# Attention with mixture of experts: the value products of a step in one group, with VectorE's and ScalarE's work around them moved

## The reference, cut to what matters

```python
def _attn_ref(q, k, v, n_sink, window):          # (2, 8, 768, 64) each, n_sink 4, window 128
    scores = scale * np.matmul(q, k.transpose(0, 1, 3, 2))
    keep = is_sink | in_window                   # 4 first keys, and the last 128 before each query
    scores = np.where(keep, scores, -1000000000.0)
    scores = scores - np.max(scores, axis=-1, keepdims=True)
    a = np.exp(scores)
    a = a / (np.sum(a, axis=-1, keepdims=True) + 1e-09)
    return np.matmul(a, v).astype(np.float32)

attn_out = _attn_ref(...)
x = attn_out.transpose(0, 2, 1, 3).reshape(B * S, H * D)   # 1536 x 512
x = _moe_ref(x=x, ...)      # each token to one of 8 experts, 192 per expert; relu(x @ w1) @ w2
return _moe2_ref(x=x, ...)  # x @ w_in, leaky relu with alpha, @ w_out
```

## Time and profile before

| | before |
|---|---|
| median of 3 runs | 635.64 us (635.63 to 636.36) |
| the profiled execution | 635.48 us, span 633.6 us |
| TensorE busy | 614.9 us (97%) |
| VectorE busy | 418.6 us (66%) |
| ScalarE busy | 308.5 us (49%) |
| GpSimd busy | 196.5 us (31%) |
| granted TensorE clock, mean of the span | 0.996 |
| the twelve attention steps until the first instruction of the routing | until 111.04 us |

### The profile page before, as it was taken

How to read it: one execution, slowest core, us unless ns; L and a number is a source line. 1 busy time by engine, 2 the same in 40 slices (tenths; PEclk the granted TensorE clock), 3 DMA queues, 4 the chain that set the end, 5 groups by cost and what they waited for, 6 DMA issues and landing times.

```text
span 633.6 us, 12921 instructions
## 1 busy us (share of the span) xinstructions
PE 614.9 (97%) x4942; PEld 554.5 (88%) x4947; DVE 418.6 (66%) x1156; ACT 308.5 (49%) x716; POOL 196.5 (31%) x211
## 2 busy tenths in 40 slices
PE   8799999889999999999999999999999999999996
PEld 4689998759899888899999888999988989999995
DVE  7788887988576979844759797439687520035552
ACT  5888884512132655532236554322566542346663
POOL 5998881010121342111113421201233410113331
PEclk9999999899999999999999999999999999999999
DMA  7477754535450242037003510360017610000001
GB/s 261 152 260 273 276 192 161 190 96 198 140 204 1 68 171 104 2 114 264 14 2 103 204 37 2 137 254 1 2 67 246 243 64 13 1 1 1 1 1 50
DMA packets 31220, 72.36 MB, mean 114 GB/s; under 512 B 2876, under 2 KB 2936, under 8 KB 31160
## 3 DMA queue, kind: packets, MB, share of 16 engines
q1 hardware_dynamic: 27232, 60.69, 27.2%
q0 software_dynamic: 1984, 6.29, 3.0%
q10 hardware_dynamic: 1944, 4.56, 1.9%
HBM read 65.22 MB, written 6.32 MB: 113 GB/s over the span
## 4 chain that ended last, share of the span: by engine, by line
PE 78%; DVE 2%; issue 0%; ACT 0%; POOLq 0%; POOL 0%; DVEq 0%
PE bank L1602 22%; PE bank L1617 21%; PE bank L1514 14%; PE bank L1505 14%; PE bank L1392 3%; PE bank L1483 1%; PE bank L1461 1%; DVE beats L971 1%; DVE beats L942 0%; PE bank L1418 0%; PE bank L1445 0%; PE bank L1233 0%; PE bank L1438 0%; PE bank L1394 0%; DVE in_slot L1055 0%
## 5 line engine op out<-in xcount | busy, mean ns | idle before, releaser
L603 POOL TENSOR_TENSOR wi_lo<-w_in,wi_hi 128x512 fp32r<-128x512 f32 x64 | 89.0, 1392 | 272.5 <-ACT wi_hi L744 272.5
L942 DVE TENSOR_SCALAR beats<-rank_row,key 128x512 bf16<-128x512 f32 (+11 forms) x144 | 92.6, 664 | 11.5 <-PE bank L1394 11.5
L1617 PE MATMUL bank<-wo_lo,g_hi 128*128 128x512 f32 x192 | 76.0, 396 | 0.0
L1617 PE MATMUL bank<-wo_hi,g_lo 128*128 128x512 f32 x192 | 75.7, 394 | 0.0
L1617 PE MATMUL bank<-wo_hi,g_hi 128*128 128x512 f32 x192 | 75.5, 393 | 0.0
L1215 DVE SCALAR_TENSOR_TENSOR g<-bank,g_neg 128x384 f32<-128x384 f32 x64 | 35.5, 555 | 52.8 <-ACT g_neg L796 52.8
L794 ACT ACTIVATE g_neg<-bank 128x384 f32<-128x384 f32 x64 | 31.4, 491 | 78.1 <-PE bank L1602 77.7
L1602 PE MATMUL bank<-y_hi,wi_hi 128*128 128x384 f32 x256 | 57.9, 347 | 0.0
L770 ACT ACTIVATE h_t<-bank 128x192 f32<-128x192 f32 x64 | 21.2, 331 | 72.8 <-PE bank L1505 72.8
L670 ACT ACTIVATE prob<-neg_s,neg_max 128x260 f32<-128x260 f32 x96 | 48.8, 509 | 15.0 <-DVE neg_max L853 12.9
L1602 PE MATMUL bank<-y_lo,wi_hi 128*128 128x384 f32 x256 | 55.2, 336 | 0.0
(11 more groups left out here) (180 smaller groups left out, 1359.6 us busy)
## 6 DMA issues: line engine op xcount, KB each, us to landing
w_a<-moe_w SPq DMA_DIRECT2D x8, 1024.0 KB, 5.1
w_a<-moe_w SPq DMA_DIRECT2D x4, 2048.0 KB, 10.3
w_b<-moe_w SPq DMA_DIRECT2D x8, 1024.0 KB, 5.1
w_b<-moe_w SPq DMA_DIRECT2D x4, 2048.0 KB, 10.2
k_raw<-k_t SPq DMA_DIRECT2D x11, 512.0 KB, 5.3
q_raw<-q_t SPq DMA_DIRECT2D x11, 512.0 KB, 4.0
w_in<-moe_w_in SPq DMA_DIRECT2D x8, 512.0 KB, 5.0
w_out<-moe_w_out SPq DMA_DIRECT2D x8, 512.0 KB, 4.5
```

Source lines behind the costliest of these rows:

```text
L603: nc.gpsimd.tensor_tensor(out=wi_lo[:, f % 2, :, :], in0=w_in[:, :, f * P:(f + 1) * P], in1=wi_hi[:, f % 2, :, :].bitcast(F32), op=ALU.sub ...
L942: return nc.vector.tensor_scalar(out=beats[:, c % 3, lo:hi], in0=rank_row[:, lo:hi], scalar1=key[:, c:c + 1], scalar2=None, op0=op)
L1617: last = nc.tensor.matmul(DOWN_BANK[t][:, :], a[:, f % 3, t * P:(t + 1) * P], w[:, f % 2, :], start=(f == 0 and n == 0), stop=(f == FC - 1 ...
```

## The change

On TensorE the products of pairs 0 and 1 no longer stand at h = 7 of a slot: all four pairs of `end` are multiplied at h = 1. On VectorE the first half of `normalise`, with the sum of the logits, moves from h = 0 to h = 1, behind the second head's maximum, and the reciprocal of the sums moves from h = 2 to h = 1. Both now stand ahead of the copy of pair 0. On ScalarE `round_next_k(front + 1)` moves from the head of the slot to behind the second exponential.

```diff
--- before.py
+++ after.py
@@ -659,8 +659,6 @@
             def attention_slot(s):
                 front, mid, end = s, s - 1, s - 2
                 for h in range(H):
-                    if h == 0 and 1 < front + 1 < STEPS:
-                        round_next_k(front + 1)
                     if front < STEPS:
                         b = front % 2
                         act.wait_ge(maxed, H * front + h + 1)
@@ -670,6 +668,8 @@
                         nc.scalar.activation(prob[b][:, h, :], neg_s[:, h % 4, :], ACT.Exp,
                                              bias=neg_max[b][:, h:h + 1], scale=-1.0,
                                              accum_out=p_sum[b][:, h, 0:1]).then_inc(exped, 1)
+                    if h == 1 and 1 < front + 1 < STEPS:
+                        round_next_k(front + 1)
                     if h == 1 and 0 <= end < STEPS:
                         act.wait_ge(pv_done, 4 * (end + 1))
                         if end:
@@ -869,7 +869,7 @@
                         if i:
                             dve.wait_ge(x_stored[b], 16 * i)
                         normalise(end, 1).then_inc(halves_read, 1)
-                    if h == 0 and 0 <= late < STEPS:
+                    if h == 1 and 0 <= late < STEPS:
                         b, i = step(late)
                         dve.wait_ge(turned, 2 * late + 2)
                         chain.after(normalise(late, 0))
@@ -877,7 +877,7 @@
                                                 axis=AX, op=ALU.add).then_inc(x_ready, 1)
                     if 0 <= mid < STEPS:
                         b, i = step(mid)
-                        if h == 2:
+                        if h == 1:
                             dve.wait_ge(exped, H * (mid + 1))
                             chain.after(nc.vector.tensor_reduce(out=p_add[:, :], in_=p_sum[b][:, :, :], axis=AX, op=ALU.add))
                             nc.vector.reciprocal(p_inv[b][:, :], p_add[:, :]).then_inc(sums_read, 1)
@@ -1345,8 +1345,8 @@
                     elif front < STEPS:
                         keep_clock(5 if h == H // 2 - 1 else 1, OT_BANK)
                     if h == 1 and 0 <= end < STEPS:
-                        values(end, 2)
-                        values(end, 3)
+                        for r in range(PAIRS):
+                            values(end, r)
                     if h == sinks_at(mid) and 0 <= mid < STEPS:
                         turn_sinks(mid)
                     if h == 4 and 0 <= end < STEPS:
@@ -1355,9 +1355,6 @@
                         sink_values(mid)
                     if h == 6 and 0 <= end < STEPS:
                         turn_and_gate(end, 0)
-                    if h == 7 and 0 <= mid < STEPS:
-                        values(mid, 0)
-                        values(mid, 1)
 
             pe.wait_ge(zeros_ready, 1)
             keep_clock(19, PT_BANK[0])
```

## The result

| | before | changed |
|---|---|---|
| median | 635.63 us (634.56 to 636.36, 4 runs) | 642.09 us (640.63 to 642.45, 4 runs) |
| ratio | | 1.0099, 95% interval 1.0077 to 1.012 |
| profiled execution | 635.48 us, span 633.6 | 640.63 us, span 638.9 |
| first instruction of the routing (L923) | 111.04 us | 116.50 us |

The change makes the kernel slower, by 6.5 us where 3.5 were forecast. The profiled execution is the fastest of the four, 1.5 us under their median. In the profiled pair all of the loss lies ahead of the routing: from L923 to the end of the span it is 522.6 us before and 522.4 after.

A forecast was written before the change was run, and what follows sets the result against it. TensorE was taken to bound slots 4 to 10; late keys would make GpSimd's chain the bound. Delays over the slots plus 0.51 at the end gave 3.63 us, so 635.48 became 639.11, forecast 639.1, range 638.0 to 640.6.

The forecast's parts named there:

- What bounds the kernel now: Slots 4 to 10: TensorE alone sets 7.61 us a slot; the rounded keys have 1.86 us of slack.
- The value products: TensorE: two of four gaps per slot go, saving 0.34 us, so its own work falls from 7.61 to 7.27.
- The rounded keys, and what follows on GpSimd: Keys end 2.19 us later, L366 starts at 3.14, next slot at 8.04 us; each slot grows by 0.43.
- VectorE, and the queues behind the waits: Moved VectorE pieces lose nothing, pair 0's copy ends at about 3.2 us; queued ScalarE and SyncE work shifts along.
- The sum for slots 2 to 4: Slot 2 starts as before at 24.54, slot 3 at +0.31, slot 4 at 40.75, +0.08 us.
- The end: Slots 11 and 12: slot 11 takes 0.34 less, slot 12's 16 products add 0.85, together +0.51 us.
- the one in which the keys are covered: Rival: L366 starts by 2.37, TensorE stays the bound, about 1.9 us saved, 633.6 us; chance 0.07.
- GpSimd was not stretched: Rival: the late start also stretches GpSimd, +0.6 us in each of eight slots, 644 us; chance 0.07.
- Nothing was made up behind the attention: Rival: the loss is made up behind the attention by a transfer as late anyway, 635.7 us; chance 0.04.

The follow-up runs named there:

- keys_back: Changed kernel with ScalarE rounding the next step's keys at the head of the slot again: 635.55 us, ratio 0.999 to the kernel before.
- group_only: Kernel before with only TensorE's value products of a step put in one group: 636.49 us, ratio 1.0008.
- keys_after_first: Changed kernel with the keys rounded behind the first exponential of a slot instead of the second: 637.81 us, ratio 1.0035 to the kernel before.
- keys_only: Kernel before with only ScalarE's rounding of the keys moved behind the second exponential: 645.29 us, ratio 1.0135.
- slot1_filled: Changed kernel with 19 unused products of zeros on TensorE in slot 1's waits: 640.79 us, ratio 1.0079 to the kernel before.
- the second (642.10 and 636.77): Changed kernel unaltered, timed again (6 runs) against 11 runs of the kernel before: 642.1 us, ratio 1.0082.
- before_look2: Third trace of the kernel before, nothing changed, taken to look for falls of TensorE's clock; L923 at 110.92 us.
- change_look3: Fourth trace of the changed kernel, nothing altered, taken for the place of the clock's fall; L923 at 115.32 us.
- change_look2: Third trace of the changed kernel, nothing altered, taken for the place of the clock's fall; L923 at 115.90 us.
- keys_back_filler: Changed kernel with keys rounded at the head of the slot and five products of zeros in slot 1: 635.71 us, ratio 0.9984 to the kernel before.
- keys_back_look: Second trace of the changed kernel with keys rounded at the head of the slot; L923 at 112.88 us.

## Why the prediction was wrong in size

*What bounds the kernel now*: right. TensorE sets 7.61 us in slots 4 to 10, and the keys had 1.86 us of slack, too little for a move by 2.19.

*The value products*: the term of 0.34 us a slot was right. It shows wherever the keys are early (7.27 block to block in keys_back and group_only).

*The rounded keys, and what follows on GpSimd*: right in mechanism and nearly in size. L366 came at 3.18 to 3.28 into a slot, and a slot took 8.10 on average for 8.04 forecast. The term was too small by 0.06 us, over seven slots 0.41. In slot 6 it lies in two hand-overs: the first maximum starts 0.64 after the slot's first load, not 0.55, and L366 starts 0.13 behind the end of the keys, not 0.06. The whole of the growth is tied to the keys' place by keys_back, keys_after_first and keys_only.

*VectorE, and the queues behind the waits*: right. The copy of pair 0 ended 3.07 us into a slot that began at 58.37, 3.2 was the bound, and no one on TensorE waited for it:

```profile
60.79 0.65 DVE L893 COPY prob_t<-bank 128x512 f32<-128x512 f32 x1
```

*The sum for slots 2 to 4* is the step that failed: it had slot 4 at 40.75, and it started at 42.11, 1.36 later. It let TensorE's work in slot 2 run as before ("Slot 2 starts as before", "Slot 4 at 40.75, against 40.67: +0.08"). It never asked what slot 1 looks like without its value products, though TensorE idled there for long already. The half clock in slot 2 is 0.97 of the 1.36, by slot1_filled. The rows that I had cited for the clock said only that it was full before, and I took that as given for the changed kernel. Another 0.13 is the execution's later start (24.67 for 24.54). The last 0.26 was an error in the sum that the trace of the kernel before could have shown: at full clock slots 2 and 3 take 16.47, the sum had 16.21. For the mask of slot 2 I took the 3.22 us of slot 4 from the end of L359 to the next L366. In slot 2 itself it is 3.47, before as in slot1_filled (32.64 to 36.11):

```profile
29.94 2.37 POOL L359 TENSOR_TENSOR q_hl<-q_raw,q_hl 64x1024 fp32r<-64x1024 f32 x1
...
35.78 2.39 POOL L366 TENSOR_TENSOR k_lo<-k_raw,k_hi 128x1024 fp32r<-128x1024 f32 x1
```

*The end*: +0.57 measured, +0.51 forecast.

Together, in the profiled pair: 1.44 + 3.45 + 0.57 = 5.46 us until L923, against 0.08 + 3.04 + 0.51 = 3.63. Without the fall and the later start it is 4.35 (101.15 against 96.80), so the sum was 0.7 too small even at full clock. The measured medians lie 6.5 us apart in the first comparison and 5.3 in the second (642.10 and 636.77). The difference between these two I take for scatter of both kernels; the last section shows where the traces scatter, but no trace is of the slower three of the first four runs. The range was too narrow for this scatter: I had built it from the chain's terms, and from three runs that lay within 0.7 us by luck.

*The rivals*: the one in which the keys are covered needed L366 by 2.37; it started at 3.2. GpSimd was not stretched (L366 2.38 us). Nothing was made up behind the attention. The Trainium skill (TensorEngine Tiling (Array Packing), Key Properties) has TensorE drained at a change of tiling mode. The traces agree in the place, with gaps of 0.17 us around each block, and merging two blocks removes two of them; that the gaps are the drain is not shown apart from their place, and they had no say in the changed kernel's time.

## What to carry to other kernels

Before moving a small piece behind waits, follow what it feeds to the end: here 1 us of work on ScalarE started a chain of 4.9 us on GpSimd, and the slack of that chain, 1.86 us, could be read from three rows. A saving on the bounding engine is worth only what the second-slowest chain leaves: with early keys GpSimd took back 0.4 us in every second slot, until its own start was moved. Work taken out of a stretch in which TensorE already idles may cost its clock; look there as well as at the path. And where one execution differs from the next by a microsecond, measure from a place behind the difference: from slot 1 to L923 traces of one program with the same clock agree to 0.03 us.

## What the runs showed of the hardware

Half clock came in stretches of 3.4 us, or twice that, and not at the same place in each execution of the same program: between 17 and 20 us in two traces of the changed kernel, between 26 and 29 in the other two. Behind the attention each trace has at least one.

Much of the scatter of all versions comes together with a late one. before_look2 had half clock from 145 to 149 us, where the first expert's products begin, and took 524.5 us from L923 to the end, where the first trace, at full clock there, took 522.6. (It had one more stretch, at 128 to 131 us; change_look3, with two stretches ahead of 140 us but none from there to 160, took 523.0.) Its stretches (144 to 148, 148 to 152), then those of the first trace:

```profile
144.00:148.00 4.00, 4.00 (x50) 3.83 (x51) 4.00 (x9) 0.91 (x3) 0.00 (x0) 0.67 1.05 398
148.00:152.00 4.00, 4.00 (x56) 3.87 (x55) 2.57 (x6) 0.66 (x2) 0.00 (x0) 0.90 0.86 322
```

```profile
144.00:148.00 4.00, 4.00 (x57) 3.87 (x54) 4.00 (x10) 0.83 (x3) 0.00 (x0) 1.00 1.01 387
148.00:152.00 4.00, 4.00 (x58) 3.87 (x57) 4.00 (x10) 0.66 (x2) 0.00 (x0) 1.00 0.80 296
```

The traces of change_look2, keys_only, group_only, keys_back_filler and keys_back_look had a fall between 144 and 157 us too, and took 524.5 to 525.1 us; the twelve traces without one took 522.4 to 523.7.
